# A weight fold with six of its eight row blocks from split operands, and later key transposes, in a fused attention and experts kernel

## The reference, cut to what matters

```python
for t in range(S):                                  # gated linear attention, 4 x 8 heads, 768 steps, 48 wide
    state = alpha[:, :, t, :, None] * state + einsum('bhd,bhe->bhde', k[:, :, t], v[:, :, t])
    y[:, :, t] = einsum('bhd,bhde->bhe', q[:, :, t], state)
x = heads of y side by side                         # 3072 tokens x 384
x = ((x @ w1) * (x @ w2)) @ w3 @ w_out              # 384 -> 1024, w3 1024 x 1024, w_out 1024 x 384
p = domain_probs / (domain_probs.sum(-1, keepdims=True) + 1e-09)
for e in range(4):                                  # experts, 384 -> 1024 -> 384
    out += p[:, e:e + 1] * (maximum(x @ we1[e], 0.0) @ we2[e])
```

## Time and profile before

| | us |
|---|---|
| median of 3 runs | 1222.52 |
| lowest, highest | 1221.64, 1222.82 |
| the profiled execution | 1221.76 |
| its span, from its first to its last instruction | 1220.0 |

### The profile page before, as it was taken

One profiled execution on the slowest core, in us unless ns is written; L12 is line 12 of the kernel. 1 busy time (PEld: TensorE's weight loads), 2 busy tenths in 40 slices (PEclk: granted clock), 3 DMA queues, 4 the chain that ended last, 5 costly groups with the idle time before them and its releaser, 6 DMA issues.

```text
span 1220.0 us, 18786 instructions
## 1 busy us (share of the span) xinstructions
PE 1215.6 (100%) x7710; PEld 1113.3 (91%) x7710; DVE 455.0 (37%) x874; ACT 275.6 (23%) x514; POOL 168.8 (14%) x148
## 2 busy tenths in 40 slices
PE   9999999999999999999999999999999999999998
PEld 6699999999999999999999999999999999999998
DVE  4897686686651121122222222221122222222222
ACT  1443233333323311111111111111111111111111
POOL 1122222222223430000000000000000000000000
PEclk9999999999999999999999999999999999999999
DMA  9743543543514341101141111123101111222201
GB/s 276 221 115 87 161 127 84 165 126 84 148 47 176 114 155 52 32 21 51 53 155 52 52 52 52 52 64 144 32 21 51 52 52 53 78 78 77 78 7 46
DMA packets 87542, 108.02 MB, mean 89 GB/s; under 512 B 38576, under 2 KB 57904, under 8 KB 86960
## 3 DMA queue, kind: packets, MB, share of 16 engines
q1 hardware_dynamic: 87184, 106.63, 28.4%
q10 hardware_dynamic: 288, 0.39, 0.1%
HBM read 86.29 MB, written 18.35 MB: 86 GB/s over the span
## 4 chain that ended last, share of the span: by engine, by line
PE 99%; DVE 0%; issue 0%; DVEq 0%
PE bank L1133 32%; PE bank L1245 25%; PE bank L984 9%; PE score_banks L1245 8%; PE bank L986 8%; PE bank L985 8%; PE bank L1023 2%; PE bank L1179 2%; PE bank L1194 1%; PE score_banks L1044 1%; PE bank L1033 1%; PE score_banks L1009 1%; PE bank L1172 0%; PE score_banks L993 0%; DVE total L962 0%; DVE inputs L727 0%
## 5 line engine op out<-in xcount | busy, mean ns | idle before, releaser
L798 DVE SCALAR_TENSOR_TENSOR h_lo<-bank,h_hi 128x512 fp32r<-128x512 f32 x192 | 132.7, 691 | 584.5 <-ACT h_hi L587 583.7
L587 ACT ACTIVATE h_hi<-bank 128x512 fp32r<-128x512 f32 x192 | 114.7, 597 | 661.7 <-PE bank L1133 661.7
L1133 PE MATMUL bank<-x_hi,we_lo 128*128 128x512 f32 x576 | 228.7, 397 | 0.0
L1133 PE MATMUL bank<-x_hi,we_hi 128*128 128x512 f32 x576 | 224.1, 389 | 0.0
L1133 PE MATMUL bank<-x_lo,we_hi 128*128 128x512 f32 x576 | 223.5, 388 | 0.0
L1245 PE MATMUL bank<-we_hi,h_hi 128*128 128x384 f32 x576 | 194.6, 338 | 0.0
L1245 PE MATMUL bank<-we_lo,h_hi 128*128 128x384 f32 x576 | 194.5, 338 | 0.0
L1245 PE MATMUL bank<-we_hi,h_lo 128*128 128x384 f32 x576 | 193.8, 337 | 0.0
L485 POOL TENSOR_TENSOR we_lo<-we_raw,we_hi (+1 forms) x48 | 60.9, 1289 | 527.8 <-ACT we_hi L548 527.8
L1133 PEld LDWEIGHTS bank<-x_lo,we_hi 128*128 128x128 f32 x576 | 108.3, 188 | 22.7
L1133 PEld LDWEIGHTS bank<-x_hi,we_lo 128*128 128x128 f32 x576 | 108.3, 188 | 22.4
(11 more groups left out here) (89 smaller groups left out, 1440.7 us busy)
## 6 DMA issues: line engine op xcount, KB each, us to landing
x_hi<-x_hi_spill SPq DMA_DIRECT2D x24, 768.0 KB, 5.0
x_lo<-x_lo_spill SPq DMA_DIRECT2D x24, 768.0 KB, 6.5
we_raw<-wset SPq DMA_DIRECT2D x4, 3072.0 KB, 10.2
inputs<-akq SPq DMA_DIRECT2D x24, 448.0 KB, 5.2
values<-v_rows SPq DMA_DIRECT2D x24, 256.0 KB, 3.9
inputs<-akq SPq DMA_DIRECT2D x24, 224.0 KB, 3.2
x_hi_spill<-x_hi_out SPq DMA_DIRECT2D x8, 576.0 KB, 5.0
x_lo_spill<-x_lo_out SPq DMA_DIRECT2D x8, 576.0 KB, 5.8
```

The lines of the kernel that those rows point to most:

```text
L587: act.activation(h_hi[:, s % 2, :], bank[s % 2][:, :], ACT.Relu).then_inc(h_hi_ready, 1)
L798: dve.scalar_tensor_tensor(out=h_lo[:, s % 2, :], in0=bank[s % 2][:, :], scalar=0.0, in1=h_hi[:, s % 2, :], op0=ALU.max, op1=ALU.subtract) ...
L1133: mm = pe.matmul(bank[s % 2][:, :], (we_hi if term < 2 else we_lo)[e % 2][:, cols], (x1_lo if term == 1 else x1_hi)[u][:, k, :], start=(i ...
```

## The change

Three things are changed.

1. In the fold's first part, row blocks `k` = 0 and 1 stay as they are. For `k` = 2 to 7 the operands are split first: ACT's `split_high(k)` copies 128x384 of `wo_sb` and 128x640 of `w3_sb` into float32r, DVE's `split_low(k)` subtracts (in place for `w3_sb`), and PE computes `split_product` from them. The new tiles lie in memory that is used later by `wb_hi` and by half of `x0`. The fold's second part keeps its float32 products.
2. On PE, `turn_keys(0, 1)` and `visit(0, 0)` now stand behind `k` = 7 (before: behind 5 and 6), `turn_keys(0, 2)` behind `n` = 5 (before: behind `k` = 7), `visit(0, 1)` behind `n` = 6 (before: 4), `turn_keys(0, 3)` behind `n` = 12 (before: 10) and `visit(0, 2)` behind `n` = 15 (before: 13).
3. The lists of ACT, DVE and SP are reordered to go with it. SP issues blocks 4 to 7 of the weights earlier among the chunk loads.

```diff
+            def split_high(k):
+                act.wait_ge(wo_loaded[k], 16)
+                act.activation(wo_hi[:, k - SPLIT_FROM, :], wo_sb[:, k, :], ACT.Copy).then_inc(split_hi, 1)
+                act.wait_ge(w3_loaded[k], 16)
+                act.activation(w3_hi[:, k - SPLIT_FROM, :], w3_sb[:, k, 0:FOLD_FIRST * P], ACT.Copy).then_inc(split_hi, 1)
...
+            for k in range(SPLIT_FROM, 5):
+                split_high(k)
             turn_keys(0, 0)
+            split_high(5)
             check(0, 0)
+            split_high(6)
+            split_high(7)
             check(0, 1)
             turn_keys(0, 1)
+            for f in range(FOLD_FIRST):
+                fold_high(f)
             x0_high(0, 0)
...
+            def split_low(k):
+                i = k - SPLIT_FROM
+                dve.wait_ge(split_hi, 2 * i + 1)
+                dve.tensor_tensor(wo_lo[:, i, :], wo_sb[:, k, :], wo_hi[:, i, :], ALU.subtract).then_inc(split_lo, 1)
+                dve.wait_ge(split_hi, 2 * i + 2)
+                at = slice(0, FOLD_FIRST * P)
+                dve.tensor_tensor(w3_lo[:, k, at], w3_sb[:, k, at], w3_hi[:, i, :], ALU.subtract).then_inc(split_lo, 1)
...
+            split_low(2)
             prepare_clamp(0, 0)
             prepare_suffixes(0, 0)
+            split_low(3)
             prepare_key_factors(0, 0)
+            split_low(4)
             prepare_query_factors(0, 0)
+            split_low(5)
             prepare_clamp(0, 1)
             prepare_suffixes(0, 1)
+            prepare_key_factors(0, 1)
+            split_low(6)
+            split_low(7)
+            prepare_query_factors(0, 1)
             advance(0, 0)
...
-            first_beside = {3: (turn_keys, 0), 4: (first_visit, 0), 5: (turn_keys, 1), 6: (visit, 0), 7: (turn_keys, 2)}
-            second_beside = {4: (visit, 1), 10: (turn_keys, 3), 13: (visit, 2)}
+            first_beside = {3: [(turn_keys, 0)], 4: [(first_visit, 0)], 7: [(turn_keys, 1), (visit, 0)]}
+            second_beside = {5: (turn_keys, 2), 6: (visit, 1), 12: (turn_keys, 3), 15: (visit, 2)}
...
+                if k < SPLIT_FROM:
+                    pe.wait_ge(wo_loaded[k], 16)
+                    pe.wait_ge(w3_loaded[k] if k else w3_first_loaded, 16)
+                else:
+                    pe.wait_ge(split_lo, 2 * (k - SPLIT_FROM) + 2)
```

More of the change, by code:

```diff
@@ L133, in gated_attention_experts @@
         scores = sb("scores", [P, 2, PAIRS, CHUNK], F32, first)
+        split = ExitStack()
+        w3_hi = sb("w3_hi", [P, FT - SPLIT_FROM, FOLD_FIRST * P], F32R, split)
+        wo_hi = sb("wo_hi", [P, FT - SPLIT_FROM, DM], F32R, split)
+        split.close()
         wb_hi = sb("wb_hi", [P, WSET], F32R, first)
@@ L141, in gated_attention_experts @@
         wp_lo = sb("wp_lo", [P, FT, DM], F32R, first)
-        x0 = [sb(f"x0_{t}", [P, CHUNKS1, KT + 1, 2, CHUNK], F32R, first) for t in range(TILES1)]
+        x0 = [sb("x0_0", [P, CHUNKS1, KT + 1, 2, CHUNK], F32R, first)]
+        split = ExitStack()
+        wo_lo = sb("wo_lo", [P, FT - SPLIT_FROM, DM], F32R, split)
+        split.close()
+        x0.append(sb("x0_1", [P, CHUNKS1, KT + 1, 2, CHUNK], F32R, first))
         x0_hi, x0_lo = [[x[:, :, :, i, :].rearrange("p c k t -> p k c t") for x in x0] for i in range(2)]
@@ L1183, in _ @@
                     pe.wait_ge(constants, CONSTANTS)
-                if k in first_beside:
-                    step, c = first_beside[k]
+                for step, c in first_beside.get(k, ()):
                     step(0, c)
```

47 lines of the change are left out of this document (26 added, 21 removed).

## The result

| | kernel before | changed kernel |
|---|---|---|
| median, 22 runs each | 1222.13 us | 1224.09 us |
| lowest to highest | 1221.49 to 1222.85 | 1222.15 to 1226.58 |
| profiled execution, span | 1221.76, 1220.0 | 1225.23, 1223.5 |

The ratio is 1.0017, with a 95% interval of 1.0011 to 1.0023: slower by 2 us. The forecast was 1224.1. What it did not say is the second row of the table: the changed kernel's runs scatter over 4.4 us, those of before over 1.4.

What follows compares the result with a forecast made beforehand. PE was taken as the bound, 99% of the chain; its 3.7 us saving was outweighed by waits on DVE, 1.6 us later net. 1221.76 + 1.6 = 1223.4, plus 0.76 for a median: 1224.1 us, range 1221.7 to 1226.7.

Steps and rivals of the forecast that it cites:

- PE's saving: Fold's first part on PE: 30 products replaced by split ones, 0.124 us less each, 3.7 us less work.
- Prices: New work: DVE subtractions 0.54 and 0.82 us, a pair 1.24 us; ACT's copies 0.43 and 0.77 us.
- Step A: Row blocks 2 and 3: loads land at 9.5 and 12.9; PE waits 0.8 and 0.85 us.
- Step B: Row blocks 4 to 7: PE doesn't wait and reaches the fold's second part at 33.3.
- Step C: DVE works 18.9 us without idling from 19.5; chunk (0, 1) masks end near 38.5; PE waits 0.9 at turn_keys(0, 2).
- Steps D and E: PE waits 0.5 us at turn_keys(0, 3), then 2.1 for fold_low(7) ahead of up1(0, 1, 0), passing 1.6 later.
- Everything behind it is shifted as it is: After PE's wait for fold_low(7): the 1.6 us delay carries unchanged to the end; nothing catches up.
- the base of the sum: Starting time: the profiled execution's 1221.76 us, with 0.76 added because the median of the runs shown lay that far above.
- dearer pairs: Rival: DVE's subtraction pairs cost up to 1.6 us, making the kernel 3.3 to 3.5 us later, 1225.9; chance 0.22.
- the last wait was not small: Rival denied here: DVE's chain behind visit(0, 2) hides, PE passes at 60.8 instead of 61.3, 1222.0; chance 0.11.
- the saving comes through: Rival: PE waits only at row blocks 2 and 3; 2.0 us less, 1220.5, or 1218.8 with early landings; chance 0.07.
- the third rival's first number: 1220.5 us, 2.0 less, if PE waits only at row blocks 2 and 3; that rival's chance was 0.07.

Runs made afterwards that it cites:

- e11: The changed kernel with all eight row blocks plain, keeping its new PE places and DVE order, without the splits' copies and subtractions: 1226.63 us, ratio 1.0034.
- e5: The changed kernel run once more, unchanged, 10 runs: 1223.32 us, ratio 1.0014 to the kernel before.
- e12: The changed kernel with its splits and new DVE order, but PE's transposes and visits at the old places: 1234.38 us, ratio 1.0106.
- e10: The changed kernel with ten matmuls of unused result on PE during its wait for fold_low(7): 1223.03 us, ratio 1.0008.
- e2: e1 with, in addition, fold_low(7) ahead of prepare_query_factors(0, 4) on DVE: 1220.64 us, ratio 0.9992.
- e7: e2 with DVE's mask(0, 1) ahead of decay_state and add_state, and one more PE wait for the state's sum: 1220.42 us, ratio 0.9985.
- e1: The changed kernel with DVE's x0_low(0, 2) moved back behind clamp and suffixes of chunk (0, 4): 1221.63 us, ratio 0.9996.

## Why the prediction came out

**PE's saving: right.** 3.7 us of work; the page shows only 2.6 us less busy time, because it adds up spans, and drains and restarts at eight waits are in them. What the splits gave back was measured at 2.3 to 3.2 us, falls of the clock included (`e11`).

**Prices: right.** The subtractions took 0.55 and 0.82, ACT's copies 0.52 and 0.72. A pair took 1.20 to 1.26 us from start to start (16.26 to 17.46 and 10.93 to 12.19 in the first trace); 1.24 had been said.

**Step A: the size was right, the landings were taken as fixed.** In the first trace the waits are 0.73 and 0.75 us from start to start (0.49 and 0.59 idle), where 0.8 and 0.85 had been said, but the blocks start at 12.33 and 15.79 and not at 11.8 and 15.3; in `e5`, where the load lands at 9.4, at 11.51 and 14.73. In the traces of the kernels that split block 2 that load landed anywhere from 7.8 (`e12`) to 10.3:

| trace | `wo_hi` 2 starts | `wo_hi` 7 starts | PE resumes | wait there |
|---|---|---|---|---|
| `e10` (same up to the resume) | 8.10 | 21.25 | 62.09 | filled, 0.18 |
| `e5` | 9.45 | 23.68 | 63.06 | 1.91 |
| first section | 10.27 | 25.36 | 64.74 | 1.90 |
| `e2` | 8.46 | 21.77 | 59.84 | none |
| `e7` | 9.11 | 22.82 | 59.83 | none |

The wait at the resume is the same for the two in which PE stood idle, and the place moves with the landings: DVE and PE move together. Block 2's landing alone doesn't set it. It is 0.8 us later in the first section's trace than in `e5`, and the resume 1.7 us: the load of block 3 was 1.2 us later (13.73 against 12.52), and that of block 7 kept DVE idle for 0.50 us, where in `e5` it kept it for none. The kernel before reads `wo_sb` at its own pace, and its scatter is 1.4 us. The forecast took one landing from one trace, 9.5, and made no range for it. The 22 runs of the changed kernel fall into four groups: fourteen at a mean clock of 1.000, ten of them from 1222.15 to 1223.63 and four from 1225.23 to 1226.07; eight at 0.999, four near 1224.3 and four near 1226.3. That the upper ones of each are late landings fits the two traces, but only these two are profiled, and `e10` had no such run in eleven.

**Step B: right in `e5`, not in the first trace.** In `e5` the second part of the fold started at 33.01 (forecast 33.3 to 33.6), with a wait of 0.23 for `fold_low(0)`. In the first trace it started at 34.67. Late landings had moved everything there, block 7's pair came late by DVE's idle time of 0.50 us, and PE waited 0.31 us for the masks of chunk 0 ahead of `turn_keys(0, 1)`, where the forecast had no wait.

**Step C: mis-sized by one term.** It left `decay_state` at its 0.33 us of the earlier trace rows. It was 1.06, and PE's wait at `turn_keys(0, 2)` was 1.69 us, or 1.96 from start to start, instead of 0.9. The forecast had looked for POOL only beside the subtractions. It was hidden in `e5`, whose masks of chunk 1 ended at 38.69 against 38.5, by DVE being on block 5 half a microsecond earlier (19.04 against 19.5; 19.04 + 18.9 + 0.73 is 38.67). In the first trace nothing hid it, and the 0.50 us of idle time came on top: 20.09 + 18.9 + 0.73 + 0.50 is 40.2, and the masks ended at 40.35. The Trainium skill, SBUF — State Buffer, section "Who interferes with whom", says that a DVE instruction with two SBUF inputs and a GpSimd instruction that reads SBUF exclude each other for a whole instruction. `decay_state` has two such inputs; it began 0.42 us behind POOL's and ended 0.21 us behind POOL's end (36.64 + 1.06 against 36.22 + 1.27), and in `e7` it took 0.36: the traces agree. The rule was quoted in the forecast and applied to one pair of instructions of two.

**Steps D and E: right.** A wait of 0.40 at `turn_keys(0, 3)` (0.5 said); `visit(0, 2)` at 49.80 in `e5` (49.6 said) and at 51.47 in the first trace; 9.64 us from `x0_low(0, 2)` to the last `fold_low` (9.6 said); 2.06 us of wait from start to start (2.1 said). From the end of the masks of chunk 1 to the end of `fold_low(7)` it is 24.3 us in all three traces of the changed kernel. `e1` and `e2` took the wait away and the time went with it.

**What the sum lacked.** "Everything behind it is shifted as it is" failed: the wait can be followed by a fall of the granted clock, which costs 1.7 us more. The forecast's 1.6 us stood for an undisturbed landing at 9.5. `e5` had that landing, and its resume was 1.75 us late. By the ends of the runs the landing is mostly earlier, though only few are profiled (the ten lowest runs centre at 1223.0, which is 0.9 above before, and `e10`, without falls, is 0.7 above), and the falls and the late landings fill the difference up to 2.0. And the base of the sum was too high. It added 0.76 us because the median of three runs lay that far above the profiled execution; over 22 runs it is 0.37. The measured difference is 1.96 us, not 1.6, and these 0.4 us cancel. That the median came out at 1224.1 is a right place and price, while the falls, the landings and the base cancel by luck. The rivals: dearer pairs did not happen; the last wait was not small; the saving comes through once that wait is gone (`e2`, `e7`), to 1220.6 and 1220.4, near the third rival's first number, 1220.5. Not tried by itself was the third part of the change, the new order of the lists of ACT and SP.

## What to carry to other kernels

When work is moved from the engine that is full to one that is nearly full, count the slack of the second at each place where the two meet, and move the instruction that waits for a third engine behind work that can be done anyway: here that one line was worth 1.5 to 2.3 us. A wait of some 2 us on PE in the middle of dense matmuls can cost nearly twice its length; look at the granted clock behind it, and compare the scatter of runs, not only the medians. And give every landing that you take from one trace a range: a load that the kernel before reads late enough becomes part of the critical chain when it must first pass through two other engines.
